# Splitting the row maximum on ScalarE and GpSimd, keeping denominators in PSUM, and summing the last two heads' rows on TensorE

## The reference

```
mask   = q_bucket[:, :, :, None] == k_bucket[:, :, None, :]
scores = where(mask, scale * q @ k.T, -1e9)
scores = scores - max(scores, axis=-1)
attn   = exp(scores);  attn = attn / (sum(attn, axis=-1) + 1e-9)
out    = attn @ v
```

## Time and profile before

| | us |
|---|---|
| median of 3 runs | 805.29 (803.74 to 806.14) |
| the profiled execution | 806.36 |
| its span (first to last instruction) | 804.5 |

### The profile page before, as it was taken

One profiled execution on the slowest core, in us unless ns is written; L12 is line 12 of the kernel. 1 busy time (PEld: TensorE's weight loads), 2 busy tenths in 40 slices (PEclk: granted clock), 3 DMA queues, 4 the chain that ended last, 5 costly groups with the idle time before them and its releaser, 6 DMA issues.

```text
span 804.5 us, 12047 instructions
## 1 busy us (share of the span) xinstructions
PE 756.5 (94%) x4086; PEld 614.3 (76%) x4086; DVE 424.7 (53%) x678; ACT 300.1 (37%) x577; POOL 329.8 (41%) x309
## 2 busy tenths in 40 slices
PE   8889999999999955989999999999999999999998
PEld 7566566666666533989999998999999888788886
DVE  7967777777876744773124122221312378336733
ACT  4457677767676431331012111101213444114411
POOL 4357877877868986339400000000003235103400
PEclk9999999999999976999999999999999999999999
DMA  3242323322221500025000000000003100010001
GB/s 83 70 105 63 77 63 79 86 70 65 72 65 50 184 1 0 1 104 211 0 1 0 0 0 0 0 0 0 1 1 140 45 1 0 14 60 6 0 13 65
DMA packets 47375, 36.11 MB, mean 45 GB/s; under 512 B 27760, under 2 KB 40048, under 8 KB 46832
## 3 DMA queue, kind: packets, MB, share of 16 engines
q1 hardware_dynamic: 46768, 32.26, 14.4%
q0 software_dynamic: 576, 3.43, 1.1%
HBM read 27.03 MB, written 3.15 MB: 38 GB/s over the span
## 4 chain that ended last, share of the span: by engine, by line
PE 73%; DVE 10%; issue 9%; POOL 6%; ACT 2%; DVEq 1%; ACTq 0%; POOLq 0%
PE PS L658 68%; DVE mneg L1352 4%; POOL esum L529 4%; DVE wgt L1381 1%; ACT ops L1079 1%; PE PS L673 1%; DVE ops L1338 1%; PE PS L771 1%; DVE ops L1321 1%; PE PS L993 1%; PE PS L939 1%; PE PS L1035 1%; PE PS L961 1%; DVE ops L1331 0%; DVE ops L1346 0%
## 5 line engine op out<-in xcount | busy, mean ns | idle before, releaser
L658 PE MATMUL PS<-ops 98*128 98x384 f32 (+1 forms) x576 | 143.5, 370 | 26.4 <-DVE mneg L1352 15.0
L658 PEld LDWEIGHTS PS<-ops 98*128 98x128 f32 (+1 forms) x576 | 94.4, 193 | 74.4 <-issue 29.2
L1549 DVE SCALAR_TENSOR_TENSOR hL<-PS,hH 128x384 fp32r<-128x384 f32 x64 | 35.7, 558 | 201.5 <-ACT hH L1240 201.5
L529 POOL TENSOR_TENSOR esum<-esum,E 128x768 f32<-128x768 f32 x64 | 119.5, 1867 | 6.8 <-ACT E L1095 5.5
L1240 ACT ACTIVATE hH<-PS 128x384 fp32r<-128x384 f32 x64 | 31.5, 492 | 227.2 <-PE PS L658 227.2
L1352 DVE TENSOR_REDUCE mneg<-PS 128x1 f32<-128x768 f32 x96 | 91.7, 956 | 30.8 <-PE PS L658 29.6
L1095 ACT ACTIVATE E<-PS 128x384 f32<-128x384 f32 x192 | 83.8, 486 | 59.7 <-PE PS L658 56.9
L658 PE MATMUL PS<-unTH,W1L 128*128 128x384 f32 x256 | 86.4, 337 | 0.0
L658 PE MATMUL PS<-unTH,W1H 128*128 128x384 f32 x256 | 86.2, 337 | 0.0
L658 PE MATMUL PS<-unTL,W1H 128*128 128x384 f32 x256 | 85.9, 336 | 0.0
L658 PE MATMUL PS<-E,vn 128*64 128x384 f32 x384 | 74.3, 509 | 8.3 <-ACT E L1095 8.3
(11 more groups left out here) (188 smaller groups left out, 1492.5 us busy)
## 6 DMA issues: line engine op xcount, KB each, us to landing
ops<-ops SPq DMA_DIRECT2D x28, 192.0 KB, 2.8
W1R<-in_moe_w_ch_dram SPq DMA_DIRECT2D x16, 256.0 KB, 2.8
W2R<-in_moe_w_ch_dram SPq DMA_DIRECT2D x4, 1024.0 KB, 6.9
qk<-in_k_dram SPq DMA_DIRECT2D x32, 96.0 KB, 2.7
qk<-in_q_dram SPq DMA_DIRECT2D x32, 96.0 KB, 3.0
vn<-in_v_dram SPq DMA_DIRECT2D x32, 96.0 KB, 2.4
out_dram<-X SPq DMA_DIRECT2D x12, 256.0 KB, 2.0
WsgR<-in_moe_w_sg_dram SPq DMA_DIRECT2D x1, 2304.0 KB, 8.4
```

What stands on the lines that cost most here:

```text
L529: pool.tensor_tensor(dst[:, :], first, A["E"][:, e_slot(t, ahead, kt), :], ALU.add).then_inc(esum_step, 1)
L658: return pe.matmul(dst, lhs, rhs, start=start, stop=stop, **kw)
L1549: dve.scalar_tensor_tensor(M1["hL"][:, f % 2, :], PS[:, f % 2, 0:HALF], 0.0, rd(M1["hH"][:, f % 2, :]), ALU.max, ALU.subtract).then_inc(hl ...
```

## The change

- The split of a head's maxima leaves VectorE. ScalarE rounds the upper part (`split_upper`), in the turn after the maxima, behind the exponentials of tile 0; GpSimd takes the lower part, nomatch and match (`split_lower`), behind the last running sum of head(-1) and ahead of the sums of v. A new semaphore, match_done, says when the comparisons are there.
- den and rec are written to PSUM, behind the sums, in the bank that holds them.
- For the last two heads (`late`) GpSimd adds no exponentials up. TensorE multiplies each tile's exponentials with 64 columns of ones, beside the products with v, into banks 4 and 5, which the maxima have left; ScalarE copies the 128x384 sums out, and `turn_back` picks the denominators from them with three products. Their exponentials don't wait for GpSimd.

```diff
+        def late(t, ahead):
+            return not t.looped and t.head(ahead) >= HEADS - 2
+        def late_bank(t, ahead):
+            return SM_BANK + t.slot(ahead, 2)
...
 # GpSimd
             def fill_head(t):
...
+                pool.wait_ge(match_done, 2 * g + 1)
...
+            def split_lower(t, ahead):
+                g, s, m = t.head(ahead), t.slot(ahead), t.slot(ahead, 2)
+                pool.wait_ge(split_hi, g + 1)
+                pool.tensor_tensor(A["mz"][:, m, :, 1], A["mneg"][:, s, :], rd(A["mz"][:, m, :, 0]),
+                                   ALU.subtract).then_inc(split_done, 1)
+                pool.tensor_scalar(A["nomatch"][:, s, :], A["mneg"][:, s, :], 0.5, 1.0, ALU.is_gt, ALU.mult).then_inc(match_done, 1)
+                pool.tensor_scalar(A["match"][:, s, :], A["mneg"][:, s, :], 0.5, 1.0, ALU.is_le, ALU.mult).then_inc(match_done, 1)
             def one_time(it, u):
-                if t.has(-1):
+                if t.has(-1) and not late(t, -1):
                     sum_exponentials(t, -1, 4)
                 if t.has(1):
+                    split_lower(t, 1)
                     sum_values(t, 0)
                     sum_values(t, 1)
-                if t.has(0):
+                if t.has(0) and not late(t, 0):
                     sum_exponentials(t, 0, 0)
...
 # TensorE, values
+                    if late(t, ahead):
+                        if kt == 0:
+                            pe.wait_ge(max_done, T * HEADS + MAX_FREE)
+                        for a in range(2):
+                            last = mm(PS[a * D:(a + 1) * D, late_bank(t, ahead), 0:HALF], ones[:, 0:D],
+                                      A["E"][:, e_slot(t, ahead, kt), half(a)], kt == 0, kt == T - 1)
 # TensorE, turn_back
+                if late(t, -1):
+                    for c in range(TH):
+                        last = mm(PS[:, SUM_BANK, DEN_AT + 2 * c:DEN_AT + 2 * c + 2], e_sum(t, -1)[:, tile(c)],
+                                  ident[:, 0:D + 1:D], True, True)
+                    last.then_inc(ot_rdy, 1)
+                    return
 # ScalarE, exponentials
-                    if a == 0 and kt <= T - 2 and (t.looped or g or kt == T - 2):
+                    if a == 0 and kt <= T - 2 and (t.looped or g or kt == T - 2) and not late(t, 0 if kt == T - 2 else -1):
                         act.wait_ge(esum_step, SUM_STEPS * (g - 1) + kt + 2 if kt < 4 else SUM_STEPS * g + 1)
 # ScalarE, raw_output
+                if late(t, -1):
+                    act.wait_ge(esum_step, SUM_STEPS * (HEADS - 2))
+                    copy(e_sum(t, -1)[:, 0:HALF], PS[:, late_bank(t, -1), 0:HALF])
...
+            def split_upper(t, ahead):
+                g, s, m = t.head(ahead), t.slot(ahead), t.slot(ahead, 2)
+                act.wait_ge(max_done, T * g + T + MAX_FREE)
+                if t.looped or g >= 2:
+                    act.wait_ge(m_rdy, 2 * g - 2)
+                copy(A["mz"][:, m, :, 0], A["mneg"][:, s, :]).then_inc(split_hi, 1)
 # ScalarE, first_times
+                split_upper(fill2, 2)
                 first_upper_halves(fill1)
                 rows_of_maximum(fill1)
                 for kt in range(T):
                     exponentials(fill0, kt)
                     if kt == 3:
+                        split_upper(fill0, 1)
                         first_upper_halves(fill0)
 # ScalarE, one_time
+                    if kt == 0 and t.has(1):
+                        split_upper(t, 1)
                     if kt == 0 and t.has(3):
                         upper_halves(t)
 # VectorE
             def maximum(t, j):
+                if j == 0 and (t.looped or g >= SLOTS):
+                    dve.wait_ge(match_done, 2 * (g - SLOTS) + 2)
...
-            def split_maximum(t):
...
             def head_output(t):
...
+                den, rec = (PS[:, SUM_BANK, at:at + T] for at in (DEN_AT + 2 * T, DEN_AT + 3 * T))
+                dve.tensor_scalar(den.rearrange("p (a c) -> p a c", a=2) if late(t, -1) else den, sums, DEN_EPS, None,
+                                  ALU.add).then_inc(norm, 1)
...
-                dve.reciprocal(A["rec"][:, :], A["den"][:, :]).then_inc(norm, 1)
+                dve.reciprocal(rec, den).then_inc(norm, 1)
                 dve.wait_ge(norm, 3 * g + 2)
-                dve.tensor_tensor(A["wgt"][:, :], A["rec"][:, :], A["match"][:, s, :], ALU.mult).then_inc(norm, 1)
+                dve.wait_ge(match_done, 2 * g + 2)
+                dve.tensor_tensor(A["wgt"][:, :], rec, A["match"][:, s, :], ALU.mult).then_inc(norm, 1)
...
-                    split_maximum(t)
...
-                if t.has(2):
-                    split_maximum(t)
```

More of the change, by code:

```diff
@@ L108, in mixer_kernel @@
                    ("mneg", [P, SLOTS, T], F32), ("nomatch", [P, SLOTS, T], F32),
-                   ("match", [P, SLOTS, T], F32), ("den", [P, T], F32), ("rec", [P, T], F32),
+                   ("match", [P, SLOTS, T], F32),
                    ("vhalf", [P, TH, D], F32), ("vsum", [P, SLOTS, D], F32), ("vmean", [P, 2, D], F32),
@@ L169, in mixer_kernel @@
         b_rdy, low_done, bits_done, mask_done, sm_rdy, max_done = sems("b_rdy low_done bits_done mask_done sm_rdy max_done")
-        split_hi, split_done, m_rdy, m_done = sems("split_hi split_done m_rdy m_done")
+        split_hi, split_done, match_done, m_rdy, m_done = sems("split_hi split_done match_done m_rdy m_done")
         st_rdy, exp_done, vsum_step, esum_step, pv_step = sems("st_rdy exp_done vsum_step esum_step pv_step")
@@ L1376, in head_output @@
                 dve.wait_ge(ot_rdy, g + 1 + TURN_FREE)
-                dve.tensor_scalar(A["den"][:, :], PS[:, SUM_BANK, DEN_AT:DEN_AT + 2 * T:2], DEN_EPS, None, ALU.add).then_inc(norm, 1)
+                sums = PS[:, SUM_BANK, DEN_AT:DEN_AT + 2 * T:2]
+                if late(t, -1):
+                    sums = PS[:, SUM_BANK, DEN_AT:DEN_AT + T].rearrange("p (c a) -> p a c", a=2)
+                den, rec = (PS[:, SUM_BANK, at:at + T] for at in (DEN_AT + 2 * T, DEN_AT + 3 * T))
+                dve.tensor_scalar(den.rearrange("p (a c) -> p a c", a=2) if late(t, -1) else den, sums, DEN_EPS, None,
+                                  ALU.add).then_inc(norm, 1)
                 dve.wait_ge(norm, 3 * g + 1)
-                dve.reciprocal(A["rec"][:, :], A["den"][:, :]).then_inc(norm, 1)
+                dve.reciprocal(rec, den).then_inc(norm, 1)
                 dve.wait_ge(norm, 3 * g + 2)
-                dve.tensor_tensor(A["wgt"][:, :], A["rec"][:, :], A["match"][:, s, :], ALU.mult).then_inc(norm, 1)
+                dve.wait_ge(match_done, 2 * g + 2)
+                dve.tensor_tensor(A["wgt"][:, :], rec, A["match"][:, s, :], ALU.mult).then_inc(norm, 1)
                 dve.wait_ge(norm, 3 * g + 3)
```

## The result

| | before | after |
|---|---|---|
| median, us | 805.41 (4 runs, 803.74 to 806.14) | 785.72 (4 runs, 785.28 to 785.90) |
| profiled execution, us | 806.36 | 785.65 |
| its span, us | 804.5 | 783.8 |

What follows compares the result with a forecast made beforehand. The loop was taken as bound by TensorE and its waits for VectorE's maxima, with holes behind it. Gains of 7.2 + 0.3 + 9.6 = 17.1 us gave a forecast of 788 us, 8 in 10 within 782 to 797.

Steps and rivals of the forecast that it cites:

- Weights in the loop: Loop of 12 heads: wgt takes 0.17 us instead of 0.84 with the reciprocal in PSUM; gain 7.2 us, bounds 5.2 and 9.6.
- The price of a PSUM source: Loop: by the skill's 120 cycles, reciprocal and wgt would each lose an estimated 0.06 us, 1.5 in all; no row shows it.
- Split in the loop: Loop: moving four operations off VectorE counts 0; ScalarE's added copy takes 0.2 us, GpSimd's three operations 0.9.
- the test: Sign of being right: from 60 to 250 us, TensorE's wait for mneg, the row maxima, is below 2 us.
- Start: Before the loop: VectorE freed of head 1's split, against ScalarE's later halves of fill1; gain +0.3 us, bounds -1 and +0.6.
- Head 14's and head 15's turns: Behind the loop: shorter folds without GpSimd's running sums (6.2 us for 9.9 and 9.0); gains 4.4 and 4.0 us.
- After it, and the transform: After head 15's turn: 0 for the turn, 1.2 us for the first transform, taking one clock fall and recovery within the transform.
- the sum: Whole kernel: 7.2 from the loop, 0.3 from the start and 9.6 from the last two heads make 17.1 us gained.
- The rival in which the clock never falls behind the loop: Last two heads and behind: full clock kept, gain 12.8 us instead of 9.6, giving 785 us; chance 0.14.
- The other rivals: Loop keeps its wait (795 us, 0.15); tail keeps holes (798, 0.08); half clock (801, 0.07); GpSimd bounds loop (822, 0.05).

Runs made afterwards that it cites:

- the last run: Changed kernel with later fold copies and 12 start products, plus later maximum copy (ScalarE), split (GpSimd) and key bits (VectorE) in the loop: 779.13 us.
- the idle additions: Changed kernel with GpSimd again making as many same-size additions in the last two heads, on other data, unread, ScalarE not waiting: 796.97 us.

## Why the prediction was right, and where its sizes were off

- *Weights in the loop.* Predicted 7.2, measured 6.24 + 0.57 for the twelfth head = 6.8. At tile 5's product the wait fell from 0.74 to 0.18, by what a head got shorter. The mechanism is shown by two runs, the addresses of den and rec alone put in (-7.8), that of rec alone taken out (+9.5, by the profile 7.0 in the loop). The prediction named den and X as its pattern; den has no SBUF input at all, and X, which has one, is the fitting one (556 to 559 ns in all 16 heads of the kernel before). The product didn't shrink: it stopped waiting for GpSimd's sum. The Trainium skill (SBUF — State Buffer, "SBUF: two separate sides") says that GpSimd's operation and one of VectorE with two SBUF inputs exclude each other for the whole instruction; wgt ending 0.02 us behind the sum agrees, and so does GpSimd's X at 270.66, which takes 2.45 us in place of 1.02 beside a fold that ends at 272.24.
- *The price of a PSUM source.* By the 120 cycles that the Trainium skill gives (VectorE: DVE Perf Modes, "The TRN2 errata") the loop would have lost an estimated 1.5 us. No run shows it: wgt at its quickest is 164 ns with one PSUM operand and 166 without; the reciprocal grew from 191 ns to 203 (rows of the kernel before and of the changed one below), not by 60.

```profile
L1379 DVE RECIPROCAL rec<-den x16: 191/191/194, 60.2 to 320.2; 128x6 f32<-128x6 f32 x16
...
L1418 DVE RECIPROCAL PS<-PS x16: 203/203/204, 60.4 to 302.0; 128x6 f32<-128x6 f32 x16
```

- *Split in the loop.* Counted at 0. The durations were right (ScalarE 0.21 for 0.2, GpSimd 0.64 for 0.9). But the count of the waits missed: I held that TensorE waits only once a head. A wait of 0.24 at tile 2's product came up beside one of 0.18 at tile 5's: 5.7 us in 24 waits, where the test said less than 2. The split's move brings them: with the split on VectorE they are 1.8 us (denominators in PSUM alone) and 1.7 (the split put back), and the move alone raised the 8.8 us in 11 waits of before to 11.6 in 22. That ScalarE's copy, ahead of the upper halves, lengthened the path over VectorE's differences fits the last run, but was not tried by itself. Alone, the move costs 1.65 us, of which 0.24 is in the loop's 11 distances; in the changed kernel it costs the loop about 0.7.
- *Start.* -0.26 measured for +0.3. The clock's fall at 42 to 45 us was in neither term, but it is in the kernel before as well (0.50 in both), so it doesn't explain the sign; what does stays open.
- *Head 14's and head 15's turns.* 5.33 less the twelfth head's 0.57 is 4.8 for 4.4, and 4.45 for 4.0; fold 6.3 for 6.2. Right, and the cause is shown by the idle additions.
- *After it, and the transform.* This is the term that was mis-sized: 0 and 1.2 predicted with one fall of the clock, 2.5 and 2.45 measured with none. These 3.7 us are the whole of the 3.6 by which the sum was short; that the four other terms cancel to within 0.2 (-0.56, -0.4, +0.4, +0.45) is luck. The bounds named for full clock (2.0 and 2.4) were close. The rival in which the clock never falls behind the loop (785) is what happened, where the prediction had taken one fall. The products with ones, weighed as a cost, help to keep it (0.86 from 275 to 300 us in the run without them), but don't ensure it: with them the clock fell to 0.93 there in the run of the last two heads alone, and to 0.71 just behind (304 to 308 us) with the split put back on VectorE.
- *The other rivals.* The loop lost most of its wait for tile 4's maximum (0.74 to 0.18), the holes shrank to 1.66 and 1.96 us, and GpSimd, 160.7 us busy of 190, still waits for exponentials (7.6 us).

## What to carry to other kernels

A tiny VectorE operation that takes several times its best duration is waiting; look at which GpSimd operation ends when it ends, and move one of its operands to PSUM rather than the work to another engine. When work leaves an engine, it lands ahead of something in another queue: place it behind what the bound engine waits for, or the wait comes back there (2.2 us here, with a step of VectorE moved as well). Short holes cost more where the clock falls in them, so a few products without use can pay (the first wgt 1.8 us earlier here).

## What the runs showed of the hardware that was not expected

- GpSimd's small operations are cheap: TENSOR_SCALAR of 128x6 in 0.25 us, where the nearest row of before had 0.42 for 128x1.
- The mean granted clock differs between runs of one kernel: without the products with ones it was 0.982 to 0.993, and the same program took 783.7 to 791.7 us; with them 0.995 to 0.997, and 785.3 to 785.9.
- Taking away a wait of TensorE didn't give its length back: 5.4 us of waits gone gave 2.3 us of loop, and the run with 1.8 us of waits (the PSUM part alone) had heads only 0.06 us closer than the one with 5.7. What else holds the loop there stays open.
